# A slot's attention in its first third, the gated steps of the same slot behind it, routing one slot behind

## The reference

```
scale = min(mag, 0.999) / (mag + 1e-6);  a = (a_re * scale, a_im * scale)
for t in range(S):
    S_re, S_im = a_re * S_re - a_im * S_im + k_t v_t^T,  a_re * S_im + a_im * S_re
    y_t = q_t @ S_re
x = (x @ w_a) * (x @ w_b) @ w_out                     # d_ff 1536
out = x;  where x @ w_skip > 0:
    e = argmax(x @ w_gate);  out += softmax(...)[e] * relu(x @ w1[e]) @ w2[e]
```

## Time and profile before

| | |
|---|---|
| median of 3 runs | 1191.31 us (1190.95 to 1192.48) |
| the profiled execution | 1189.92 us, span 1188.1 us |
| TensorE busy | 907.3 us, 76% |
| VectorE busy | 818.9 us, 69% |
| ScalarE busy | 368.9 us, 31% |
| GpSimd busy | 248.9 us, 21% |
| mean granted clock of TensorE | 0.91 of full |

### The profile page before, as it was taken

The page is one execution under the profiler, slowest core; times in us unless marked ns, Lnnn a source line. Parts: engine busy times, 40 slices in busy tenths (PEclk is TensorE's granted clock), DMA queues, the critical chain, the costliest instruction groups (busy, mean ns, idle before and its releaser), DMA issues. The chain is left out here.

```text
span 1188.1 us, 15277 instructions
## 1 busy us (share of the span) xinstructions
PE 907.3 (76%) x5652; PEld 809.2 (68%) x5652; DVE 818.9 (69%) x1375; ACT 368.9 (31%) x650; POOL 248.9 (21%) x188
## 2 busy tenths in 40 slices
PE   0002335997988899888889989889999992199997
PEld 0001335876877788767778878787888881199997
DVE  4986998799599889939987996997110004266672
ACT  4013103513522441342136135213222211154551
POOL 0515103112211311221141123114111113501001
PEclk9999665999989999888999989899999995599999
DMA  8211304002300410230141023001011117457650
GB/s 239 63 36 44 126 0 113 27 22 72 107 28 21 133 55 21 67 108 20 28 133 47 21 72 109 27 21 47 28 28 47 34 33 278 155 200 238 206 193 22
DMA packets 47949, 97.15 MB, mean 82 GB/s; under 512 B 4774, under 2 KB 39096, under 8 KB 47872
## 3 DMA queue, kind: packets, MB, share of 16 engines
q1 hardware_dynamic: 31632, 72.91, 19.5%
q10 hardware_dynamic: 13680, 18.68, 5.7%
q0 software_dynamic: 2560, 4.51, 1.0%
HBM read 83.70 MB, written 15.77 MB: 84 GB/s over the span
## 5 line engine op out<-in xcount | busy, mean ns | idle before, releaser
L812 POOL TENSOR_TENSOR s_gsb<-s_asb,s_bsb 128x384 f32<-128x384 f32 x96 | 105.6, 1100 | 621.1 <-ACT s_bsb L481 621.1
L238 PE MATMUL ps<-s_wo,s_gsb 128*128 128x384 f32 x576 | 203.9, 490 | 4.8 <-issue 4.8
L260 PE MATMUL ps<-s_qk 48*128 48x128 f32 x384 | 49.3, 341 | 177.6 <-DVE s_qk L679 105.4
L260 PEld LDWEIGHTS ps<-s_qk 48*128 48x128 f32 x384 | 37.5, 236 | 182.1 <-issue 107.1
L238 PEld LDWEIGHTS ps<-s_wo,s_gsb 128*128 128x128 f32 x576 | 108.0, 191 | 56.5 <-issue 6.1
L227 PE MATMUL ps<-s_xh,s_wah 128*128 128x384 f32 x288 | 83.9, 403 | 21.6 <-ACT s_bsb L481 10.8
L479 ACT COPY s_asb<-ps 128x384 f32<-128x384 f32 x96 | 45.9, 478 | 95.9 <-PE ps L227 95.9
L227 PEld LDWEIGHTS ps<-s_xh,s_wah 128*128 128x128 f32 x288 | 51.9, 210 | 29.6 <-ACT s_bsb L481 14.0
L481 ACT COPY s_bsb<-ps 128x384 f32<-128x384 f32 x96 | 46.2, 481 | 78.4 <-PE ps L227 78.4
L227 PE MATMUL ps<-s_xl,s_wah 128*128 128x384 f32 x288 | 69.7, 352 | 0.0
L227 PE MATMUL ps<-s_xh,s_wal 128*128 128x384 f32 x288 | 67.3, 342 | 0.0
(11 more groups left out here) (181 smaller groups left out, 2140.9 us busy)
## 6 DMA issues: line engine op xcount, KB each, us to landing
s_wo<-in_w_out ACTq DMA_DIRECT2D x95, 192.0 KB, 2.4
e_w1s<-in_w SPq DMA_DIRECT2D x8, 1536.0 KB, 7.1
e_w2s<-in_w SPq DMA_DIRECT2D x8, 1536.0 KB, 7.3
s_gre<-in_are_t SPq DMA_DIRECT2D x8, 672.0 KB, 7.2
s_gim<-in_aim_t SPq DMA_DIRECT2D x8, 672.0 KB, 5.3
s_qk<-in_k_t SPq DMA_DIRECT2D x8, 672.0 KB, 7.6
s_qk<-in_q_t SPq DMA_DIRECT2D x8, 672.0 KB, 5.4
s_vt<-in_v_t SPq DMA_DIRECT2D x8, 576.0 KB, 6.8
```

What stands on the lines that cost most here:

```text
L238: mm = pe.matmul(ps[:, DOWN + t, 0:DM], gsb[:, n % 2, t * P:(t + 1) * P], wo[:, n % WO_BUFS], start=(n == 0), stop=(n == NF1 - 1))
L260: mm = pe.matmul(ps[:, SC + v, pr * CH:(pr + 1) * CH], lanes(kf, pr, j, v), lanes(qf, pr, j, v), start=(c == 0), stop=(c == 1))
L812: pool.tensor_tensor(gsb[:, x % 2], asb[:, x % 2], bsb[:, x % 2], ALU.mult).then_inc(s["g_ready"], 1)
```

## The change

The loop has 9 slots. In slot u the first four steps (LEAD = 4) are the last four gated steps, 8 to 11, of slot u - 1, and the whole attention of slot u, all three chunks, lies among them, between halves of the ups. Behind them come the first eight gated steps of slot u itself. `rows_out` of slot u - 1 stands after the first four steps, and its three routings at steps 5 to 8, one slot behind. Slot 8 holds four gated steps and the last routing. ScalarE and VectorE follow: the halves of `root`, `newton`, `inverse` and `scale` are placed one by one among the three chunks, `blocks` (rounds, totals and carry), `spreads` and `last` (norm and both factors) come behind `low_part(2)`; `state` is cut in `added` and the rest; `squares2` and `inverse2` stand behind `gate(10, 1)`, ahead of `gate(11, 0)`. GpSimd's `keys` stand behind the product of step 11. SP loads the keys and queries of slot u + 2 ahead of storing rows. `up` takes a half (x = 0 or 1), `gate` is ScalarE's copy of that half.

```diff
 WO_BUFS = 3
+LEAD = 4
...
@@ -177,23 +178,24 @@
 
             def slot(b, par):
                 u, static = number(b, par)
-                if not static or u >= 2:
+                if not static or u < NU - 2:
+                    sp.wait_ge(s["kt_ready"], 6 * (u + 1))
+                    load_keys(u + 2, par)
+                    sp.wait_ge(s["y_ready"], CU * (u + 1))
+                    load_queries(u + 2, par)
+                if not static or u >= 1:
 
                     for t in range(CU):
-                        n = CU * (u - 2) + t
+                        n = CU * (u - 1) + t
                         sp.wait_ge(s["o_copied"], n + 1)
                         row = n * P
                         dst = out[row:row + P] if static else out[bass.ds(row, P)]
                         sp.dma_start(dst, x1[:, t]).then_inc(s["st_out"][t], 16)
                 if not static or u < NU - 2:
-                    sp.wait_ge(s["kt_ready"], 6 * (u + 1))
-                    load_keys(u + 2, par)
-                    sp.wait_ge(s["y_ready"], CU * (u + 1))
-                    load_queries(u + 2, par)
                     sp.wait_ge(s["q_made"], 4 * (u + 2))
                     load_real(u + 2, par)
 
-            slots_of(slot, NU + 1)(sp)
+            slots_of(slot, NU)(sp)
...
-                has_gated = not static or 1 <= u <= NU
-                has_route = not static or u >= 2
-                w, r = u - 1, u - 2
+                has_last = not static or u >= 1
...
+                def up(n, x):
+
+                    if not (has_att if n >= LEAD else has_last):
+                        return
+                    g, f, of = NF1 * u + n - LEAD, (n - LEAD) % NF1, par if n >= LEAD else 1 - par
+                    if f == 0 and x == 0:
+                        pe.wait_ge(s["x_split"], CU * (u + 1))
+                    if static and u == 0:
+                        pe.wait_ge(s["w_split"], 2 * (f // (NF1 // 4) + 1 + 4 * x))
+                    at_least("ab_copied", 2 * g - 1 + x)
+                    wh, wl, bank, done = ((wah, wal, UP_A, "up_a"), (wbh, wbl, UP_B, "up_b"))[x]
+                    products = [(w_, x_, c) for w_, x_ in ((wh, xh), (wh, xl), (wl, xh)) for c in range(KC)]
+                    for i, (w_, x_, c) in enumerate(products):
+                        mm = pe.matmul(ps[:, bank, 0:TG], w_[:, c, f * P:(f + 1) * P], x_[:, of, c],
+                                       start=(i == 0), stop=(i == len(products) - 1))
+                    mm.then_inc(s[done], 1)
+
+                def down(n):
+
+                    if not (has_att if n >= LEAD else has_last):
+                        return
+                    g, f = NF1 * u + n - LEAD, (n - LEAD) % NF1
+                    pe.wait_ge(s["g_ready"], g + 1)
+                    pe.wait_ge(s["ld_wo"][f % WO_BUFS], 16 * (NF1 // WO_BUFS * u + (n - LEAD) // WO_BUFS + 1))
+                    if f == 0:
+                        at_least("o_copied", CU * u)
                     for t in range(CU):
                         mm = pe.matmul(ps[:, DOWN + t, 0:DM], gsb[:, n % 2, t * P:(t + 1) * P],
-                                       wo[:, n % WO_BUFS],
-                                       start=(n == 0), stop=(n == NF1 - 1))
+                                       wo[:, f % WO_BUFS],
+                                       start=(f == 0), stop=(f == NF1 - 1))
                     mm.then_inc(s["down_done"], 1)
...
+                        at_least("xr_copied", CU * (u - 1))
+                        if not static or u >= 2:
+                            pe.wait_ge(s["lg_copied"], CU * (u - 1) + 1)
...
+                    if t == 0:
+                        pe.wait_ge(s["u_added"], 2 * CU * (u + 1) if has_att else 2 * CU * NU)
...
-                for n in range(NF1):
-                    j, m = n // 4, n % 4
-                    if n == 0:
-                        if has_route:
-                            down(w - 1, NF1 - 1)
-                        if has_gated:
-                            up(0)
-                    elif has_gated:
-                        up(n)
-                        down(w, n - 1)
-                    if has_route and n in (4, 8):
-                        route_logits(j - 1)
-                    if m == 0 and has_att:
-                        scores(j)
-                        turn_keys(j, 0)
-                    if m == 1:
-                        if has_att:
-                            turn_keys(j, 1)
-                        if has_route:
-                            route_turn(j)
...
+                if has_att:
+                    scores(0)
+                    turn_keys(0, 0)
+                up(0, 0)
+                if has_att:
+                    turn_keys(0, 1)
+                up(0, 1)
+                if has_att:
+                    adds(0)
+                    values(0)
+                down(-1)
+                if has_att:
+                    turn_values(0)
+                up(1, 0)
+
+                if has_att:
+                    scores(1)
+                    turn_keys(1, 0)
+                up(1, 1)
+                if has_att:
+                    turn_keys(1, 1)
+                down(0)
+                if has_att:
...
+                if has_att:
+                    scores(2)
+                    turn_keys(2, 0)
+                down(1)
+                if has_att:
+                    turn_keys(2, 1)
+                up(3, 0)
+                if has_att:
+                    adds(2)
+                    values(2)
+                up(3, 1)
+                if has_att:
+                    turn_values(2)
+                down(2)
+
+                down(3)
+                for n in range(LEAD, NF1):
+                    up(n, 0)
+                    up(n, 1)
+                    if n > LEAD:
+                        down(n - 1)
+                    t = n - LEAD - 1
+                    if has_last and 1 <= t <= CU:
+                        route_logits(t - 1)
+                    if has_last and 0 <= t < CU:
+                        route_turn(t)
...
+                act.wait_ge(s["mag2"], 2 * w + i + 1)
+                mark(act.activation(tp[L, 1, x], tp[L, 0, x], ACT.Ln))
+                after(w, 2 * i + 1)
+                mark(act.activation(tp[L, 1, x], tp[L, 1, x], ACT.Exp, scale=-0.5))
+                after(w, 2 * i + 2)
+                act.activation(gim[L, par, 0, x], tp[L, 1, x], ACT.Square).then_inc(s["y0"], 1)
...
-            PREP_AT = ((0, "first"), (0, "behind"), (1, "behind"), (8, "before"), (8, "behind"))
...
+                def gate(n, x):
+                    if not (has_att if n >= LEAD else has_last):
+                        return
+                    g, f = NF1 * u + n - LEAD, (n - LEAD) % NF1
+                    if x == 0:
+                        at_least("g_ready", g - 1)
+                    act.wait_ge(s[("up_a", "up_b")[x]], g + 1)
+                    act.copy((asb, bsb)[x][:, n % 2], ps[:, (UP_A, UP_B)[x], 0:TG]).then_inc(s["ab_copied"], 1)
+                    if x == 1 and (has_att or f < NF1 - 1):
+
+                        nxt = (f + 1) % NF1
+                        at_least("down_done", g + 1 - (WO_BUFS - 1))
+                        act.dma_start(wo[:, nxt % WO_BUFS], w_out[nxt * P:(nxt + 1) * P])\
+                           .then_inc(s["ld_wo"][nxt % WO_BUFS], 16)
...
+                prep(squares)
+                if has_att:
+                    keys(0, 0)
+                gate(0, 0)
+                prep(root, 0)
+                if has_att:
+                    keys(0, 1)
+                gate(0, 1)
+                if has_att:
+                    values(0)
+                prep(root, 1)
+                if has_att:
+                    high_part(0)
+                gate(1, 0)
+
+                if has_att:
+                    keys(1, 0)
+                prep(inverse, 0)
+                gate(1, 1)
+                if has_att:
+                    keys(1, 1)
+                    values(1)
+                gate(2, 0)
+                if has_att:
+                    high_part(1)
+                prep(inverse, 1)
+                gate(2, 1)
+
+                if has_att:
+                    keys(2, 0)
+                    keys(2, 1)
+                gate(3, 0)
+                if has_att:
+                    values(2)
+                gate(3, 1)
+                if has_att:
+                    high_part(2)
+
+                if has_last:
+                    rows_out()
+                for n in range(LEAD, NF1):
+                    gate(n, 0)
+                    gate(n, 1)
+                    t = n - LEAD - 1
+                    if has_last and 1 <= t <= CU:
+                        logits(t - 1)
+                    if has_last and 0 <= t < CU:
+                        turned(t)
+                    if n == NF1 - 2:
+                        prep(squares2)
+                        prep(inverse2)
...
                 magnitude()
                 masked(0)
```

(34 more changed lines are left out.)

230 lines of the change are left out of this document (87 added, 143 removed).

## The result

| | kernel before | changed kernel |
|---|---|---|
| median of the runs | 1191.16 us (1190.95 to 1192.48, 4 runs) | 1233.51 us (1232.65 to 1238.59, 4 runs) |
| ratio, 95% interval | | 1.0362 [1.0346, 1.0378] |
| span of the profiled execution, granted clock | 1188.1 us, 0.913 | 1230.8 us, 0.899 |

A forecast was written before the change was run, and what follows sets the result against it. No engine alone bound the kernel: full slots of 103.5 us were chains through VectorE, ScalarE and TensorE. Expert start 105.4 + 7 x 113.8 + 123.3 = 1025.3 against 987.8, 37.5 more on 1189.9, plus 1.4: 1229 us, range 1205 to 1262.

The forecast's parts named there:

- the 6 that were named as a sign of being wrong: Before squares2: ScalarE waiting over 6 us for the second spread would mean VectorE's route is mis-sized.
- A: Slots preparing another: preparation stays hidden, period stays at 103 us, 1153 us in all; chance 0.10.
- B: Slots preparing another: saved fill and boundary waits cancel, period 108.2 to 108.8, 1189 to 1194 us; chance 0.03.
- the break-even: Length of a slot that prepares another at which the expert stage starts as before: 108.4 us.
- rival C: Slot start: TensorE stays at 1.2 GHz until some 28 us in, period above 118.5, over 1262 us; chance 0.07.
- the front: First part of a slot on TensorE: 4 ups, 5 downs, 3 attention chunks, head's loss and a root wait, 53.2 us.
- GpSimd's products: VectorE's stretch of blocks: seven GpSimd products collide with its instructions, costing 0.6 x 7 = 4.2 us.
- products that hold VectorE for their whole length: VectorE's stretch of blocks: seven products of 1.16 us each block it fully; period 3.9 longer, time 27 us more.
- The hand-overs and the product ahead of the keys: End of the preparation: step 11's GpSimd product 1.0 us and a dozen hand-overs between engines 1.3, together 2.3 us.
- The two routes: Slot start to squares2: VectorE's through low part and blocks 90.4 us, TensorE's through ups, downs and attention 89.8 us.
- The head's loss: Slot start to values(0) on TensorE: 7.9 us lost against unstalled full clock, 6.1 waits and 1.8 clock.
- The tail: After the seven preparing slots: slot 7's work 93, remaining steps 22.5 and routing 7.8, together 123.3 us.

The follow-up runs named there:

- e1: Changed kernel with squares2 and inverse2 one gated step earlier, behind gate(9, 1): 1233.37 us, 1.034 of the kernel before.
- e2: Changed kernel with 5 rounds of blocks in place of 7 in slots 1 to 7, part of the computation left out: 1205.75 us, 1.012 of the kernel before.
- e3: Changed kernel with squares2 and inverse2 one gated step earlier and two rounds of blocks left out: 1198.51 us, 1.004 of the kernel before.
- e6: Changed kernel with 96 idle matmuls, never read, in TensorE's gap at each slot's end: 1240.03 us, 1.040 of the kernel before.
- c3: Changed kernel with squares' input landed a slot earlier, GpSimd's factors on VectorE, idle matmuls in gaps and slot 0: 1202.58 us, 1.010 of the kernel before.
- e8: Changed kernel with the squares' input landed a slot earlier and TensorE's gap closed by three groups of idle matmuls: 1213.70 us, 1.021 of the kernel before.
- e7: Changed kernel with the squares' input landed a slot earlier and 96 idle matmuls in each gap: 1221.37 us, 1.025 of the kernel before.

## Why the prediction was right, and where its terms were off

The forecast was 1229 us from seven slots of 113.8; measured are 1233.5 us and six slots of 114.0 and one of 122.7. The rows that it named for itself are there: gaps before the scores ended by the last query factor, the second squares waiting for VectorE, the old chain beside the gated steps turned into an idle TensorE. Two came in another size. The gaps were to be 12 to 18 us long, from a chain of 21.1 us less an up and a down of 5.1, and are 18.2 to 24.3: the chain takes 21.9, and the second squares, at which it begins, wait less than 3 us for the spread in slots 1, 3 and 5 only (2.75) and 4.7 to 5.4 in slots 2, 4 and 6. In slot 0 that wait is 8.9 us, beyond the 6 that were named as a sign of being wrong.

**The mechanism: shown.** TensorE's 21.8 busy us of 22 beside the end of the preparation became 4.3 of 22, and a factor for which it had never waited between slots now holds it up seven times. Shortening the end by 4.1 us took 4.0 from each slot of the changed kernel. The measured period excludes A and B, which needed a period under 108.8. Two rounds less of work and an earlier end together brought it to 108.6 and the time to 1.004 of before, which is where the prediction put the break-even, 108.4.

**Start.** The last factor of slot 0 was made at 103.1, 2.3 us earlier than the 105.4 of the earlier trace rows. In the profiles of the changed kernel and of e1, e2, e3 and e6, which share all instructions up to there, that moment lies between 103.1 and 104.2, with the second squares at 82.0 to 83.1 (84.26 in the kernel before): what moves it was not looked into.

**Slot 0, mis-sized by 8.9 us.** It was put at 113.8 like the rest and took 122.7. The third low part came 58.0 us into it, not 50.7, and the blocks and the end took 42.8 and 21.9. Its chunks have no gated step of a slot before among them, so TensorE is never full there; its groups of the scores still take 0.64 us at 128.16, far behind the head, and of the matmuls with the carried state those of the second chunk take 1.06 us and those of the third 1.91:

```profile
128.16 0.64 PE L270 MATMUL ps<-s_qk 48*128 48x128 f32 x4
...
139.04 1.06 PE L305 MATMUL ps<-s_zst,s_gim 112*128 112x96 f32 x8
...
156.66 1.91 PE L305 MATMUL ps<-s_zst,s_gim 112*128 112x96 f32 x8
...
160.59 0.56 DVE L787 TENSOR_TENSOR s_xl<-ps,s_xh 128x384 fp32r<-128x384 f32 x1 [7.60 <-ACT s_xh L504]
```

It is what rival C said of the half clock, in one slot of seven. How much it weighs, e1, e2, e3 and e6 show, whose instructions in this stretch are the same: there the second chunk ran at half clock too (1.91 us), and the third low part came 62.1 to 62.4 us into the slot, 4 later. c3, whose idle matmuls kept the clock up, had it 52.9 us behind its first scores, where the changed kernel needs 57.9, although the idle matmuls took TensorE's time as well. That the half clock makes the whole difference isn't shown. And the miss is small by luck: the sum gave slot 0 the four ups and five downs of the front (22.5 us), which it doesn't have, and left out the half clock beyond the head. Two errors of opposite sign made 7.3 us in the front.

**Slots 1 to 6, right to 0.2 us by terms that are off.** That they cancel so well is luck. By the marks of slots 1 to 6 the third low part ends 50.3 us into the slot (predicted 50.7), from there to the second squares are 41.8 us (predicted 34.2 + 1.3 + 4.2 = 39.7), and from there to the last factor 21.9 (predicted 21.1 + 2.3 = 23.4). So the stretch of blocks was 2.1 us short. The term is that of GpSimd's products: in slot 1 VectorE works without a pause from the low part to the spread, 40.5 us for what takes 34.2 where nothing collides, so the seven products, 8.9 us long together, cost it nearly all of 6.3 us and not 4.2. That lies between the prediction's value and its case of products that hold VectorE for their whole length (8.1). The hand-overs and the product ahead of the keys were 1.5 too long, since only 0.8 of the 2.3 appeared; and 0.4 in the front. Within the front, the copy of values(0) came at 16.4 us on the mean (14.9 to 18.3), 2.4 earlier than the 18.8 of the prediction, and the two chunks behind it took that back. In the even slots the first chunk has no state carried into it, and their front is 2.2 us shorter (49.2 us against 51.4); `state(2)`, which only they have, makes the stretch behind it 2.6 longer (43.1 against 40.5). The prediction had told only the second apart, and took it at its mean.

**The two routes.** They were put 0.6 us apart, VectorE's being the later. e2 confirms the order and puts TensorE's 3.9 us below, so VectorE's route of 90.4 was 1.7 too short (92.1) and TensorE's of 89.8 some 1.6 too long (88.2).

**The half clock.** The head's loss was 6.1 for waits and 1.8 for the clock. With the waits as they are in the changed kernel, shortening the half clock by a part changed nothing. With the landing out of the way and the clock full through the head, 1.9 to 2.4 us went in the slots where nothing else was in the way (1.3 on the mean of e8). So the 1.8 was about right as the price of the clock by itself, and too much as a term of this sum, since the landing of 5.1 us lies beside it. In the changed kernel as it stands a full clock for the scores was reached in one slot (slot 6 of e6), and gave nothing; a full clock over its whole head was not measured.

**The tail.** 121.9 us against 123.3: slot 7 and its steps were 1.4 us shorter, and the expert stage another 1.4.

The sum of these is -2.3 + 8.9 + 1.4 (six slots of 114.0 for 113.8) - 1.4 = 6.6 us at the start of the expert stage, 1031.9 against 1025.3. The expert stage gives 1.4 of it back and the distance from span to median 0.5, which leaves the 4.5 us between 1229 and 1233.5 but for rounding. The one term that mattered is slot 0.

## What to carry to other kernels

Before a piece of work is moved to fill an idle stage, look up what it covers where it stands: eight gated steps went into an idle stage of TensorE, and what they left behind is a serial chain of 22 us on VectorE and ScalarE, uncovered in each of seven slots. Busy sums (93 and 87.5 us of 103.5) did not show this, one window over the chain did, in which TensorE was busy for 21.8 of 22 us. And a helper engine that shares the work of the critical one is worth measuring: here two engines needed 5.1 us for the four products that one does in 3.6. And what idle work is to gain is read slot by slot: the mean of e7 said nothing, while two of its slots, in which the clock stayed up, were 2.4 us shorter.
